# Sin, Square and the gating of a pair of hidden tiles, issued behind that pair's own copies and turn

## The reference

```
# per head, chunk of 32 queries, keys = 8 memory + 16 left + 32 + 8 right
a = exp(scores - max); a = a / (sum(a) + 1e-9);  out[chunk] = a @ v_full
x = out as (3072 tokens, 512)
h = x @ w_in                       # 512 -> 2048
g = h * np.cos(h)
x = g @ w_out                      # 2048 -> 512
h = max(x @ w1, x @ w2, x @ w3)    # 512 -> 768, three times
return h @ w_out2                  # 768 -> 512
```

## Time and profile before

| | us |
|---|---|
| median of 3 runs | 1004.38 (1004.29 to 1008.68) |
| the profiled execution | 1003.52, its span 1001.7 |
| block 3 of the first stage (179.13 to 224.67) | 45.54 |
| block 7, no attention work (about 358 to 392) | pairs 4.16 apart |
| granted TensorE clock, mean | 0.983 |

### The profile page before, as it was taken

The page is one execution under the profiler, slowest core; times in us unless marked ns, Lnnn a source line. Parts: engine busy times, 40 slices in busy tenths (PEclk is TensorE's granted clock), DMA queues, the critical chain, the costliest instruction groups (busy, mean ns, idle before and its releaser), DMA issues.

```text
span 1001.7 us, 18402 instructions
## 1 busy us (share of the span) xinstructions
PE 962.1 (96%) x7564; PEld 933.3 (93%) x7564; DVE 675.9 (67%) x926; ACT 516.0 (52%) x689; POOL 210.2 (21%) x231
## 2 busy tenths in 40 slices
PE   5989999999999999999999999999999999999998
PEld 4878889898989899989999999999999999999998
DVE  4355666566665568997998989866736546577761
ACT  1586786867778788333433334543323224444441
POOL 3341111112121212100100000662100000584610
PEclk6799999999999999999999999999999999999999
DMA  9983656574653434443445434432020031324532
GB/s 223 227 212 101 185 149 187 145 201 129 192 165 111 149 131 155 149 145 125 149 145 172 148 106 133 140 120 92 32 95 32 33 127 48 121 95 146 192 116 84
DMA packets 65395, 135.41 MB, mean 135 GB/s; under 512 B 5920, under 2 KB 27424, under 8 KB 65312
## 3 DMA queue, kind: packets, MB, share of 16 engines
q1 hardware_dynamic: 54944, 98.58, 34.2%
q0 software_dynamic: 10368, 35.66, 10.8%
HBM read 87.03 MB, written 47.19 MB: 134 GB/s over the span
## 4 chain that ended last, share of the span: by engine, by line
PE 73%; ACT 10%; DVE 9%; DMA 4%; issue 3%; POOL 1%; SPq 1%; DVEq 0%; ACTq 0%
PE ps L595 23%; PE ps L597 22%; PE ps L596 22%; PE ps L611 2%; DVE work L1178 2%; ACT work L901 2%; PE ps L636 2%; DVE units L1215 2%; ACT work L896 1%; ACT work L903 1%; PE ps L645 1%; DMA early_qk<-qk_in 1%; DVE ssum L1145 1%; ACT work L893 1%; ACT work L872 1%
## 5 line engine op out<-in xcount | busy, mean ns | idle before, releaser
L595 PE MATMUL ps<-units 128*128 128x384 f32 (+1 forms) x1940 | 611.1, 315 | 8.3 <-DVE units L1215 2.0
L597 PE MATMUL ps<-units 128*128 128x384 f32 (+1 forms) x1940 | 602.9, 311 | 0.0
L596 PE MATMUL ps<-units 128*128 128x384 f32 (+1 forms) x1940 | 602.6, 311 | 0.0
L595 PEld LDWEIGHTS ps<-units 128*128 128x128 f32 x1940 | 369.4, 190 | 20.2 <-issue 6.9
L596 PEld LDWEIGHTS ps<-units 128*128 128x128 f32 x1940 | 369.6, 191 | 0.0
L597 PEld LDWEIGHTS ps<-units 128*128 128x128 f32 x1940 | 369.2, 190 | 0.0
L921 ACT CAST units<-work 128x1024 fp32r<-128x1024 f32 x96 | 85.7, 939 | 123.9 <-DVE work L1201 106.6
L1076 ACT COPY work<-ps 128x384 f32<-128x384 f32 (+1 forms) x144 | 63.6, 454 | 146.9 <-PE ps L597 146.8
L1173 DVE SCALAR_TENSOR_TENSOR work<-work 128x768 f32<-128x768 f32 x64 | 62.2, 972 | 71.8 <-ACT work L896 71.8
L1215 DVE TENSOR_TENSOR units<-work,units 128x1024 fp32r<-128x1024 f32 x96 | 102.1, 1105 | 12.2 <-ACT units L921 12.2
L486 POOL DMA_DIRECT2D g_dram<-work x64 | 46.8, 731 | 291.4 <-DVE work L1178 286.7
(11 more groups left out here) (96 smaller groups left out, 845.4 us busy)
## 6 DMA issues: line engine op xcount, KB each, us to landing
g_dram<-work POOLq DMA_DIRECT2D x64, 384.0 KB, 3.3
work<-g_dram SPq DMA_DIRECT2D x48, 512.0 KB, 3.7
work<-qk_in SPq DMA_DIRECT2D x36, 384.0 KB, 5.3
work<-v_in SPq DMA_DIRECT2D x40, 256.0 KB, 5.0
work<-w_in POOLq DMA_DIRECT2D x40, 256.0 KB, 3.6
h_dram<-work SPq DMA_DIRECT2D x24, 384.0 KB, 2.9
work<-h_dram SPq DMA_DIRECT2D x18, 512.0 KB, 3.9
work<-y_dram SPq DMA_DIRECT2D x8, 768.0 KB, 6.5
```

The lines of the kernel that those rows point to most:

```text
L595: pe.matmul(o, wh, mh, start=start, stop=False, skip_group_check=onto)
L596: pe.matmul(o, wh, ml, start=False, stop=False, skip_group_check=onto)
L597: return pe.matmul(o, wl, mh, start=False, stop=stop, skip_group_check=onto)
```

## The change

Both loops issue the second half of a pair's work at once instead of one pair later.

```
-                        if i:
-                            cosine(i - 1)
+                        cosine(i)
...
-            cosine(TILES - 1)
...
                         turn(i)
-                        if i:
-                            gated(i - 1)
+                        gated(i)
...
-            gated(TILES - 1)
```

## The result

The changed kernel took 1032.98 us (median of 4 runs, 1030.89 to 1034.34) against 1006.17 before (4 runs in that comparison); ratio 1.026, 95% interval 1.023 to 1.030. Slower, as forecast, and inside the range, 7 us above the 1026 named. The profiled execution took 1032.86, 29.3 more than that of before.

What follows compares the result with a forecast made beforehand. PE, busy 96% of the span, was taken to bound the kernel, standing behind a chain through ACT and DVE. Terms: -1.0 + 7.4 + 3.1 + 12.7 = 22.2 us on 1003.52, 1025.7, named as 1026; range 1011 to 1035.

Steps and rivals of the forecast that it cites:

- the cost of one pair: Undisturbed pair: ACT stands 1.20 us for the turn, DVE 1.78 for Sin and Square; evacuation to evacuation 4.31 against 3.11.
- about 1.1 us, some 55 times: Sign in the new profile: ACT waits this long before nearly each Sin for DVE's turn, where no such wait stood.
- term B: Second `turn_out` of blocks 1 to 5: 0.78 us later each; 3.1 us for blocks 2 to 5.
- rival 1: Whole kernel: spare time of ACT and DVE covers the new waits, no change, 1003.5 us; chance 0.06.
- Term A: Head of blocks 2 to 6, Exp ahead of the last evacuation: first `turn_out` 1.48 us late, 7.4 us in five blocks.
- Term C: Block 7 and the way into the second stage: pairs too dense for the new chain, 12.7 us lost, bounds 5 and 16.
- Term D: Blocks 0 and 1: stores go out sooner, a gain, sum -1.0 us, bounds -4.3 and +2.3.
- The clock: PE's two new gaps in block 7 may each bring half-rate work worth 1 to 2 us; up to 4 in the range only.
- 2: Rival: stores release buffers a pair sooner, block 0's waits of 2.52 and 1.80 us go, 999.2 us; chance 0.06.
- 3: Rival: only the last block pays, ACT catches up at the heads of blocks, 1015 us; chance 0.14.
- 4: Rival: more than followed, with Term C at 16, the clock 4 and Term D at +2.3, 1036 us; chance 0.14.

Runs made afterwards that it cites:

- experiment 3: Changed kernel, with only the gating of the first pair of blocks 1 to 6 issued behind sums and normalise: 1022.7 us, ratio 1.0175.
- the fill: GpSimd fills w_in's low parts with zeros instead of subtracting: 1028.82 us (again 1028.59) on the changed kernel, 1005.37 us on the kernel before.

## Why the prediction was right, and where it was not

**What bounds the kernel, and the cost of one pair.** Right for an undisturbed pair: ScalarE waits 1.09 or 1.10 us for the turn in 30 of the 56 cases, VectorE 1.78 or 1.79 for Square in 56 of 64. In 20 more ScalarE waits 2 to 4 us, in a steady block twice, 3.4 and 3.2, where sums, shift and `normalise` stand ahead of the turn (203.71 and 216.25 in block 3); "about 1.1 us, some 55 times" had left those out, though the walk in term B has them. Spare time on average (the rule of the busiest engine, rival 1) covered nothing, since the lists are worked in order.

**Term A.** Right in size (block 6, which has A alone, cost 1.49 for 1.48; PE's wait at the first `turn_out` grew by 0.7 us and that for the copy by 0.4) and in its cause, which experiment 3 shows: one gating ahead of the sums.

**Term B.** Too small: blocks 2 to 5 cost 2.54 on average and not 2.26, so with A at 1.48 B was 1.06 and not 0.78. They alternate; every other one waits 1.03 us instead of 0.65 at the second `turn_out`. What makes them alternate was not followed up.

**Term C.** 13.5 for 12.7. The evacuations of block 7 came 0.2, 2.4, 3.1, 7.2, 7.1, 9.6, 12.4 and 13.7 late beside block 6; walked were 0.3, 2.6, 3.3, 7.5, 7.4, 9.9, 11.1 and 12.4. The step is at the seventh. The chain of waits there shows why, in the changed kernel and before:

```profile
406.43 5.64 DMA work<-g_dram
```

```profile
382.61 3.78 DMA work<-g_dram
```

I had the transfer at 3.8; VectorE waited 2.14 us for it. It now starts right behind two loads of weights (issued at 405.35), which before were issued only at 385.43, as it ended; that they slowed it is likely and not tested. The stands came elsewhere than walked: 4.53 for 4.8, then 0.33 (at 412.27) where I had 3.1, then 4.46 for 3 at the entry of the second stage. The sum held because ScalarE and VectorE set it, not PE.

**Term D.** The step that failed: "`values` comes 1.0 earlier and the first `turn_out` 2.0 earlier". `values` seemed to (61.59 for 62.56), but by luck: in this execution the first evacuation was 1.6 sooner (38.17 for 39.78), and counted from it `values` came 0.6 later. `turn_out` came at 70.33, 0.6 later by the span's time. I had walked the turns at 0.96 and the denominators at 0.18. The trace of before showed 1.96 and 1.92 for pair 3's turn and the denominators, beside GpSimd's subtraction; pair 1's turn it showed at 0.96, but with the gating at once that one meets a subtraction too (2.45). Before, ScalarE did not wait for its pair's turn, and now it does. That is 1.49 (pair 1) + 1.35 (pair 3) + 1.27 (denominators, which held the old order as well) = 4.1 us. PE, having stood 4.97, then ran at 1.2 GHz for the next slices:

```profile
68.00:72.00 4.00, 1.67 (x9) 1.67 (x9) 3.02 (x4) 0.84 (x2) 1.11 (x1) 0.58 1.01 288
72.00:76.00 4.00, 4.00 (x22) 3.75 (x24) 1.65 (x2) 2.41 (x6) 2.52 (x3) 0.57 0.13 48
```

The granted clock is 0.58 and 0.57, and the second `turn_out` is late by 2.4 us more (79.91 - 70.33 = 9.58 for 7.22). Together 6.5; from the first evacuation on, block 0 was 4.6 behind where 1.8 ahead was walked, 6.4 apart. The 1.6 us of the sooner start hid a part of that in the table. With the fill, block 0 is 1.9 ahead by the same count, as walked.

**The clock.** I had granted it up to 4 us in block 7, where PE waits anyway. Around both gaps it fell to 0.50, for 6.8 us each: 3.4 us a piece where I had said 1 to 2. The trace shows that none of it was PE's to lose there: no evacuation of block 7 waited for PE, and the slow slices only filled the stand of 3.1 that I had walked; behind the second gap PE still waited 0.30 us for VectorE's low part at 444.02, 30.0 after the same matmul of before (414.01), and the low parts themselves are 30.0 later. In block 0, where I had not looked for it, it counted. Before, the clock had also fallen there, from 63 to 67, behind the 2.52 us of the earlier trace rows.

**The rivals.** 2, faster by the sooner stores: the stores' waits did go, as it said, and it decided at `turn_out`, where PE waited more, not less. 3 was wrong, since A and B were paid. 4 was right that D could end above my sum, and it ended even above its bound of 2.3 (4.1); but C was 13.5, not 16, and the clock took nothing in block 7. That the whole came to within 7 us of the 1026 rests on A, B and C, and in part on the sooner start, which is luck.

## What to carry to other kernels

Moving an instruction closer behind what it needs turns a wait that was over into one that an in-order engine stands for, and everything queued behind stands too: price it by what is next in that list, not by the engine's busy share. Engines need not be moved together: here Sin at once where matmuls leave time made the kernel 7 to 8 us faster, of which 0.4 us a block are surely the order's; gating at once costs, and both cost where pairs come as fast as the chain is long. When a step joins the critical path, look up its slowest rows, not its usual length.

## What the runs showed of the hardware

A 128x768 operation of VectorE with two inputs took 1.18 to 2.46 us instead of 0.96 where it met GpSimd's subtraction of two tiles at its start, and a 128x24 addition of a constant 1.45 to 1.93 instead of 0.18. The first ended 0.82 or 0.83 us after the subtraction in all ten places, the second 0.04 or 0.05 after it in all eleven.

After PE had stood for 4.5 to 5.3 us, its granted clock went to 0.50 (1.2 GHz) in all 13 places in the traces, for 6.8 us in eight of them and 3.4 us in five. After shorter stands it went both ways: for 3.4 us after the 2.52 us in block 0 of the kernel before, after 2.33 us in blocks 5 and 6 of the changed order without block 7, and not at all after the 2.24 to 2.33 us in blocks 1 to 6 of the changed kernel.
